# A chunk's second 64 outputs in exchanged halves of the partitions, so that the products with the states use all four quarters of TensorE's array

## What is computed

```python
for t in range(S):
    cur = np.einsum('bhd,bhe->bhde', u[None] * kt, vt)
    y[:, :, t] = np.einsum('bhd,bhde->bhe', rt, state + cur)
    state = wt[:, :, :, None] * state + np.einsum('bhd,bhe->bhde', kt, vt)
```

## Time and profile before

| | us |
|---|---|
| median of 3 runs (612.76 to 614.74) | 613.3 |
| the profiled execution | 613.21 |
| its span on the core | 611.5 |
| PE busy / DVE busy / ACT busy | 588.1 / 327.2 / 267.1 |
| PE busy from 85 to 510 us | 424.68 of 425 |

### The profile page before, as it was taken

The page is one execution under the profiler, slowest core; times in us unless marked ns, Lnnn a source line. Parts: engine busy times, 40 slices in busy tenths (PEclk is TensorE's granted clock), DMA queues, the critical chain, the costliest instruction groups (busy, mean ns, idle before and its releaser), DMA issues.

```text
span 611.5 us, 15134 instructions
## 1 busy us (share of the span) xinstructions
PE 588.1 (96%) x6342; PEld 526.4 (86%) x6342; DVE 327.2 (54%) x710; ACT 267.1 (44%) x540; POOL 12.4 (2%) x30
## 2 busy tenths in 40 slices
PE   7888989999999999999999999999999999999983
PEld 6787989899989999999899999999999999997433
DVE  8768675476755654566266635564455323323304
ACT  3845543544453344433543354335433346553314
POOL 4000000000000000000000000000000000000000
PEclk9989999999999999999999999999999999999996
DMA  8975602324402330333023312323031097667628
GB/s 292 348 229 174 183 25 77 101 62 117 124 18 86 100 101 1 101 88 88 29 62 100 101 41 61 83 67 93 2 101 28 14 366 266 218 228 277 230 82 309
DMA packets 46309, 77.50 MB, mean 127 GB/s; under 512 B 3296, under 2 KB 35040, under 8 KB 43664
## 3 DMA queue, kind: packets, MB, share of 16 engines
q1 hardware_dynamic: 45040, 71.80, 37.8%
q0 software_dynamic: 1200, 4.72, 2.5%
HBM read 67.46 MB, written 9.04 MB: 125 GB/s over the span
## 4 chain that ended last, share of the span: by engine, by line
PE 86%; DMA 6%; DVE 4%; issue 2%; ACT 1%; SPq 0%; DVEq 0%; ACTq 0%
PE hps L1262 32%; PE acc L1397 31%; DMA w2s<-w 2%; PE yps L1215 2%; PE mps L1293 2%; PE zps L1195 2%; PE mps L1469 2%; PE zps L1206 2%; DMA stage<-w_out 1%; PE zps L1215 1%; PE zps L1221 1%; DMA raw<-dmaj 1%; DMA out<-obuf 1%; PE mps L1482 1%; PE mps L1502 1%
## 5 line engine op out<-in xcount | busy, mean ns | idle before, releaser
L1102 DVE TENSOR_TENSOR gl<-g,gh 128x384 fp32r<-128x384 f32 (+1 forms) x144 | 74.0, 514 | 232.8 <-ACT gh L802 232.5
L1262 PE MATMUL hps<-xh,wi_hi 128*128 128x384 f32 (+1 forms) x432 | 147.7, 342 | 2.3 <-DVE xl L499 2.1
L1262 PE MATMUL hps<-xh,wi_lo 128*128 128x384 f32 (+1 forms) x432 | 137.3, 318 | 0.0
L1262 PE MATMUL hps<-xl,wi_hi 128*128 128x384 f32 (+1 forms) x432 | 137.3, 318 | 0.0
L1397 PE MATMUL acc<-wo_hi,gh 128*128 128x384 f32 x384 | 129.8, 338 | 0.6 <-ACT x L809 0.3
L1397 PE MATMUL acc<-wo_hi,gl 128*128 128x384 f32 x384 | 129.6, 338 | 0.0
L1397 PE MATMUL acc<-wo_lo,gh 128*128 128x384 f32 x384 | 129.6, 338 | 0.0
L802 ACT ACTIVATE gh<-g 128x384 fp32r<-128x384 f32 (+1 forms) x144 | 70.4, 489 | 130.8 <-PE acc L1397 130.4
L798 ACT ACTIVATE g<-hps 128x384 f32<-128x384 f32 (+1 forms) x144 | 65.7, 456 | 133.5 <-PE hps L1262 130.8
L1262 PEld LDWEIGHTS hps<-xh,wi_hi 128*128 128x128 f32 x432 | 81.4, 188 | 12.7 <-issue 6.6
L1262 PEld LDWEIGHTS hps<-xl,wi_hi 128*128 128x128 f32 x432 | 81.8, 189 | 0.9
(11 more groups left out here) (235 smaller groups left out, 733.8 us busy)
## 6 DMA issues: line engine op xcount, KB each, us to landing
raw<-dmaj SPq DMA_DIRECT2D x23, 903.0 KB, 5.6
w1s<-w SPq DMA_DIRECT2D x16, 768.0 KB, 6.4
w2s<-w SPq DMA_DIRECT2D x16, 768.0 KB, 6.3
vn<-vnat SPq DMA_DIRECT2D x24, 192.0 KB, 2.6
tests<-wall SPq DMA_DIRECT2D x6, 768.0 KB, 15.2
out<-obuf SPq DMA_DIRECT2D x12, 384.0 KB, 4.2
y_scratch<-ybuf SPq DMA_DIRECT2D x44, 96.0 KB, 2.0
x<-y_scratch SPq DMA_DIRECT2D x22, 192.0 KB, 2.5
```

Source lines behind the costliest of these rows:

```text
L1102: dve.tensor_tensor(out=gl[F % 2][:, 0:wide], in0=g32[F % 2][:, 0:wide], in1=gh[F % 2][:, 0:wide].bitcast(fp32), op=ALU.subtract).then_inc ...
L1262: last = pe.matmul(hps[F % 2][:, 0:wide], w[:, g, at:at + 128], v[i % 2][:, g, 0:wide], start=m == 0, stop=m == 3 * G - 1)
```

## The change

Results of the second 64 tokens (c = 1) go to the exchanged half of the partitions: head par 0 to partitions 64 to 111, par 1 to 0 to 47. `out_rows` gives the place. With it a `from_state` product takes quarter (par, par) for c = 0 and (par, 1 - par) for c = 1, and a `from_block` product (c, par) for c = 0 and (1, 1 - par) for c = 1. Since `ybuf` then holds the second 64 columns exchanged, all that reads or writes it goes by halves: the bonus sums (a second set of weights with exchanged columns, `heads_u[1]`, `headsum[1]`), the values (the host exchanges them in `dmaj`), the stores to DRAM (four DMAs of 64 columns for two of 128), `permute` (a second `place_rows`). Counts of semaphores follow. In `outputs` the order becomes: for each pair the two products whose result another quarter continues (`apart`), then the two others (`same`); then `from_block` of `same` for pair 0, the wait, and the rest.

```diff
+        def out_rows(c, par):
+
+            at = HALF * (par if c == 0 else 1 - par)
+            return slice(at, at + D)
...
                 for par in range(2):
-                    sp.dma_start(view[par], ybuf[n % 2][HALF * par:HALF * par + D]).then_inc(y_stored[n % 2], 16)
+                    for c in range(2):
+                        cols = slice(HALF * c, HALF * (c + 1))
+                        sp.dma_start(view[par][:, :, cols], ybuf[n % 2][out_rows(c, par), :, cols]).then_inc(y_stored[n % 2], 16)
...
-            pool.memset(place_rows[:, :], 0.0).then_inc(made, 1)
+            for c in range(2):
+                pool.memset(place_rows[c][:, :], 0.0).then_inc(made, 1)
...
-            for par in range(2):
-                rows = place_rows[HALF * par:HALF * par + D]
-                pool.affine_select(out=rows, in_=rows, compare_op=ALU.not_equal, fill=1.0, base=96 + D * par,
-                                   pattern=[[-1, 288]], channel_multiplier=1).then_inc(made, 1)
+            for c in range(2):
+                for par in range(2):
+                    rows = place_rows[c][out_rows(c, par)]
+                    pool.affine_select(out=rows, in_=rows, compare_op=ALU.not_equal, fill=1.0, base=96 + D * par,
+                                       pattern=[[-1, 288]], channel_multiplier=1).then_inc(made, 1)
...
-                for p in range(HP):
-                    last = act.activation(heads_u[p][:, :], headsum_f[:, :], ACT.Copy, scale=ucols[:, p:p + 1])
+                for c in range(2):
+                    for p in range(HP):
+                        last = act.activation(heads_u[c][p][:, :], headsum[c][:, :].bitcast(fp32), ACT.Copy,
+                                              scale=ucols[:, p:p + 1])
...
-            dve.tensor_copy(headsum[:, :], headsum_f[:, :])
+            dve.tensor_copy(headsum[0][:, :], headsum_f[:, :])
+            dve.tensor_copy(headsum[1][:, 0:D], headsum_f[:, HALF:R])
+            dve.tensor_copy(headsum[1][:, D:HALF], headsum_f[:, D:HALF])
+            dve.tensor_copy(headsum[1][:, HALF:R], headsum_f[:, 0:D])
...
-                    return pe.matmul((zps, yps)[c][rows, p * HALF:(p + 1) * HALF], (state[n % 2], midway)[c][rows, p, :],
+                    return pe.matmul((zps, yps)[c][out_rows(c, par), p * HALF:(p + 1) * HALF], (state[n % 2], midway)[c][rows, p, :],
...
-                for swap in (1, 0):
-                    for p in range(HP):
-                        for par in range(2):
-                            last = from_state((par + swap) % 2, par, p)
-                    if swap:
+                apart, same = ((0, 1), (1, 0)), ((0, 0), (1, 1))
+
+                for p in range(HP):
+                    for c, par in apart:
+                        last = from_state(c, par, p)
+                    if p == HP - 1:
                         last.then_inc(crossed, 1)
+                    for c, par in same:
+                        from_state(c, par, p)
+                for c, par in same:
+                    from_block(c, par, 0)
                 pe.wait_ge(crossed, n + 1)
                 for p in range(HP):
-                    for c in range(2):
-                        for par in range(2):
-                            last = from_block(c, par, p)
+                    for c, par in apart:
+                        last = from_block(c, par, p)
+                    if p + 1 < HP:
+                        for c, par in same:
+                            from_block(c, par, p + 1)
...
-                for g, p in ((0, 0), (0, 1), (1, 1), (1, 2), (2, 2), (2, 3)):
-                    at = 96 + 128 * g - 96 * p
-                    last = pe.matmul(hps[c][:, g * C:(g + 1) * C], place_rows[:, at:at + 128], ybuf[c][:, p, :],
-                                     start=p == g, stop=p > g)
+                for half in range(2):
+                    cols = slice(HALF * half, HALF * (half + 1))
+                    for g, p in ((0, 0), (0, 1), (1, 1), (1, 2), (2, 2), (2, 3)):
+                        at = 96 + 128 * g - 96 * p
+                        last = pe.matmul(hps[c][:, g * C + HALF * half:g * C + HALF * (half + 1)], place_rows[half][:, at:at + 128],
+                                         ybuf[c][:, p, cols], start=p == g, stop=p > g)
...
                 for p in range(HP):
-                    last = pe.matmul(bonus_bank(n)[0:R, p * C:(p + 1) * C], heads_u[p][:, :], ruk[n % 2][:, p, :],
-                                     start=True, stop=True)
+                    for c in range(2):
+                        last = pe.matmul(bonus_bank(n)[0:R, p * C + HALF * c:p * C + HALF * (c + 1)], heads_u[c][p][:, :],
+                                         ruk[n % 2][:, p, HALF * c:HALF * (c + 1)], start=True, stop=True)
...
-                        pe.matmul(mps[0:R, :], headsum[:, :], rukh[:, :, :].rearrange("d p t -> d (p t)"),
-                                  start=True, stop=False)
-                        pe.matmul(mps[0:R, :], headsum[:, :], rukl[:, :, :].rearrange("d p t -> d (p t)"),
-                                  start=False, stop=True).then_inc(u_done, 1)
+                        for c in range(2):
+                            cols = slice(HALF * c, HALF * (c + 1))
+                            sums = mps[0:R, :].rearrange("e (p t) -> e p t", p=HP)[:, :, cols]
+                            pe.matmul(sums, headsum[c][:, :], rukh[:, :, cols], start=True, stop=False)
+                            last = pe.matmul(sums, headsum[c][:, :], rukl[:, :, cols], start=False, stop=True)
+                        last.then_inc(u_done, 1)
```

More of the change, by code:

```diff
@@ L116, in attention_mlp_soft_experts @@
         headsum_f = sb("headsum_f", [R, R])
-        headsum = sb("headsum", [R, R], f32r)
+        headsum = [sb(f"headsum{c}", [R, R], f32r) for c in range(2)]
         ucols = sb("ucols", [R, HP])
@@ L132, in attention_mlp_soft_experts @@
         strip = place[0] - 2 * G * ST * 4 + 2 * C * 4
-        heads_u = [sb(f"heads_u{p}", [R, R], at=strip + (p + 1) * ST * 4) for p in range(HP)]
+        heads_u = [[sb(f"heads_u{c}{p}", [R, R], at=strip + (HP * c + p + 1) * ST * 4) for p in range(HP)] for c in range(2)]
         g32 = [sb(f"g32_{i}", [128, ST]) for i in range(2)]
         gh = [sb(f"gh{i}", [128, ST], f32r) for i in range(2)]
-        place_rows = sb("place_rows", [R, 288], at=place[0])
+        place_rows = [sb(f"place_rows{c}", [R, 288], at=place[0] + c * 288 * 4) for c in range(2)]
         gl = [sb(f"gl{i}", [128, ST], f32r) for i in range(2)]
@@ L405, in general_loads @@
                 for par in range(2):
-                    sp.dma_start(ybuf[n][HALF * par:HALF * par + D], view[par]).then_inc(gen_back, 16)
+                    for c in range(2):
+                        cols = slice(HALF * c, HALF * (c + 1))
+                        sp.dma_start(ybuf[n][out_rows(c, par), :, cols], view[par][:, :, cols]).then_inc(gen_back, 16)
         def split_x(act, i, c):
@@ L693, in _ @@
             pool.memset(ident[:, :], 0.0).then_inc(made, 1)
[L694 removed]
+            for c in range(2):
+                pool.memset(place_rows[c][:, :], 0.0).then_inc(made, 1)
             for q in range(EG):
                 pool.memset(sel[q][:, :, :], 0.0).then_inc(made, 1)
[L697 removed]
+            pool.wait_ge(made, 6 + EG)
             for c in range(2):
@@ L712, in _ @@
                 for j in range(4):
-                    pool.wait_ge(made, 10 + EG + 4 * q + j)
+                    pool.wait_ge(made, 13 + EG + 4 * q + j)
                     s0 = SPE * (4 * q + j)
@@ L1029, in start_up @@
                 products(0)
-                dve.wait_ge(made, 10 + EG)
+                dve.wait_ge(made, 13 + EG)
                 for m in range(3):
@@ L1318, in start_up @@
             def start_up():
-                pe.wait_ge(made, 10 + EG)
+                pe.wait_ge(made, 13 + EG)
                 pe.wait_ge(headsum_made, 1)
@@ L1592 @@
             dmaj[:, HALF * par:HALF * par + D, q, :, 1:] = by_feature(a)[:, par]
+    for par in range(2):
+        dmaj[:, HALF * par:HALF * par + D, VV, :, 1 + HALF:] = by_feature(v)[:, 1 - par, :, :, HALF:]
     ucol = np.zeros((R, HP), np.float32)
```

17 lines of the change are left out of this document (9 added, 8 removed).

## The result

| | before | after |
|---|---|---|
| median, us | 612.76 (7 runs, 611.89 to 614.74) | 617.47 (7 runs, 615.62 to 622.83) |
| the profiled execution, us | 613.21 | 615.69 |
| its span, us | 611.5 | 614.0 |
| PE busy / DVE busy / ACT busy, us | 588.1 / 327.2 / 267.1 | 591.9 / 327.2 / 268.3 |

The changed kernel is slower: its time over that of before is 1.0088, with a 95% interval of 1.0067 to 1.0109. The forecast was 614.6 us with a range that ended at 617.5, so the time lies just inside its end, and "slower by over 0.3%" had 0.41. Run again beside other kernels, the same file gave 617.63 us against 613.18 (1.0109, 1.0072 to 1.0147).

What follows compares the result with a forecast made beforehand. PE was taken to bound 85 to 510 us, and one PE, DVE and ACT chain the start-up; 613.2 + 4.05 (start-up) + 0.7 (chunk 3 sums) - 0.2 (later sums) - 3.15 (`outputs`) gave 614.6 us, range 610.0 to 617.5.

Steps and rivals of the forecast that it cites:

- The outputs: In `outputs`, first to last start falls from 1.33 to 1.18 us: 0.15 us gained a chunk, 3.15 us for 21 chunks.
- Rival (A): In `outputs`, two row halves writing one PSUM bank take turns, so it lasts 1.56 us: 623.0 us; chance 0.07.
- Rival (C): In `outputs`, the wait for `crossed` costs nothing, so the gain is the full 0.41 us a chunk: 608.9 us; chance 0.05.
- (D): In the stores, packets of 256 bytes take twice the time, `x` comes late and ACT stands: about 617.5 us; chance 0.06.
- The narrow products with full weights: In `permute` and `bonus_sums`, weight loads set the step, so half-width passes cost +1.3 us per `permute`, +0.7 per sums.
- Rival (B): In `permute` and the bonus sums, weight load is not the limit and half the width costs half: 610.1 us; chance 0.08.
- The start-up up to `xh`: Start-up chain through the second `permute`: 0.9 + 0.7 + 1.3 - 0.15 + 1.3 = 4.05 us later.
- So the shift is whole: At the start-up's end, the first slot waits for ACT's tests, so all 4.05 us of delay carries through.
- the sums of chunk 3: Bonus sums in the start of the steps: not hidden by any PE wait, +0.7 us.
- the sums of chunk 2: Bonus sums in step 0: their +0.7 us is hidden by PE's waits of 0.29 and 0.88 us for DVE.
- The sum: Whole kernel, against the profiled 613.2 us: + 4.05 + 0.7 - 0.2 - 3.15 = +1.4, so 614.6 us.
- the sums of the later chunks: Head sums as four products of 256 columns for two of 512: 0.46 us for 0.47, -0.2 us over 20 chunks.

Runs made afterwards that it cites:

- sums_away: The changed kernel with the second head-sum matrix (`headsum[1]`) allocated behind all other buffers, so every other buffer lies where it lay before; measured 617.82 us.

## Why the prediction was wrong, point by point

The forecast was 1.4 us more than before and the medians are 4.7 us apart. Three things make the difference: where the new buffer lies, which the sum didn't have; how much of the start-up's cost reaches the end, which it had too high; and executions at a lower clock, which it didn't have.

**The outputs**: right. The gain was forecast as 0.15 us a chunk with a wait of 0.30 us; it is 0.178 with a wait of 0.28 to 0.29. That is 21 x 0.03 = 0.6 us more than in the sum, inside its bounds.

**Rival (A)**, two row halves in one bank: ruled out. Four passes start every 0.056 us in `from_state` after the change, with both row halves writing into `zps` and both into `yps`. The rule of the Trainium skill that was weighed there (TensorEngine Tiling (Array Packing), Gotcha 1: PSUM Pressure) is not borne out where the two write different partitions. Rival (C), a wait that costs nothing, falls by the gap from 138.54 to 138.70; (D) by `x`, which still lands in a median of 2.5 us, with the stores at 1.7 for 2.0:

```profile
y_scratch<-ybuf SPq DMA_DIRECT2D x88, 48.0 KB, 1.7
x<-y_scratch SPq DMA_DIRECT2D x22, 192.0 KB, 2.5
```

**The narrow products with full weights**: right. The weights set the step, not the width: 0.113 us for `permute` (0.114 forecast), 0.10 us for the sums ((1.78 - 0.27) / 15 in the rows above, 0.098 forecast). Rival (B) falls.

**The start-up up to `xh`**: 3.93 us for 4.05 forecast, though not link by link: `score` came 0.47 us later and the sums of chunk 0 cost 0.7, those of chunk 1 next to nothing.

**"So the shift is whole"**: the first step that failed. Of 3.93 us at 28 us only 2.42 were left at the first mark (95 us), where the sum had 4.75 with the sums of chunk 3, less 0.15 for that chunk's outputs. Where it went, the starts of the same product with `w_in` before and after show: the first one starts 3.93 us later after the change, the first behind PE's branch at the start-up's end 3.17. The branch had more idle time before than after:

```profile
34.55 0.39 PE L1372 MATMUL acc<-warm 128*128 128x256 f32 x1 [1.43 <-issue]
```

```profile
37.73 0.39 PE L1398 MATMUL acc<-warm 128*128 128x256 f32 x1 [0.69 <-issue]
```

Behind the sums of chunk 2 the shift is 3.46 us, and some ten us of PE's work later it is 1.49. Before:

```profile
48.30 0.36 PE L1262 MATMUL hps<-xh,wi_hi 128*128 128x256 f32 x1
...
60.00 0.37 PE L1262 MATMUL hps<-xh,wi_hi 128*128 128x256 f32 x1
```

After:

```profile
51.76 0.36 PE L1285 MATMUL hps<-xh,wi_hi 128*128 128x256 f32 x1
...
61.49 0.36 PE L1285 MATMUL hps<-xh,wi_hi 128*128 128x256 f32 x1
```

Between these two lie PE's waits of 0.29 and 0.88 us for DVE; neither is in the profile after. The prediction let them swallow the 0.7 us of the sums of chunk 2 and nothing else. The stretch swallowed 1.97 us: their 1.17, the 0.18 won in the outputs of chunk 2, and some 0.6 that I can't assign. Of the 2.2 us that the sum has too much up to the first mark, 0.74 are the branch's and 1.27 this stretch's. I asked of ACT and the first slot whether they had slack, and not of the slots behind.

The profiled execution of before had a stretch at a low clock right there, which the profile after doesn't have:

```profile
36.00:40.00 4.00, 4.00 (x20) 4.00 (x19) 4.00 (x5) 2.62 (x5) 0.49 (x1) 0.57 0.91 238
```

It isn't what makes the shift small: none of the profiles of the other kernels with this start-up has such a stretch, and their first marks lie on both sides of its 95.33 us (94.69 to 96.37).

**"The sum"**: the second step that failed, and the dear one. Between the marks the forecast has 19 x 0.15 + 0.2 = 3.05 us of gain; they show 0.31. The term that is missing is where the new matrix lies: nothing in the sum asked what it does to the buffers behind it. Its price is 2.9 us in the kernel before and 3.1 us (386.49 - 383.39) in the changed one, 0.5 of it in the sums of the later chunks, which the prediction had at -0.2 us and which took 0.67 more. In the profiled execution, +1.4 us forecast and +2.5 measured, the errors nearly cancel, which is luck: 4.6 - 2.4 = 2.2 us too much up to the first mark, 3.05 - 0.31 = 2.7 too little between the marks, and behind the second, where the sum had a gain of 0.15, 0.4 us of loss, 0.5 too little.

**The clock**: what the profiled execution could not show. The forecast took the median to lie where the profiled execution lay, as before the change (0.1 us). After it the median is 1.8 us above, since some executions are 4 to 8 us longer at a lower mean clock, and the runs with parts of the change put this on the halved permutes. One row of before bears on it, and I passed over it: right behind the branch it has already a stretch at a low clock (the row of 36 to 40 us above).

So the mechanism in `outputs` was read rightly, and so was the price of the narrow products in `permute` and in the sums of chunk 0. What failed is what becomes of a cost on its way to the end, and a cost that no instruction carries. With 64 bytes more behind the new matrix the changed kernel takes 613.71 us, 0.9 us from the forecast, and that nearness is luck in part: all but one of its executions at a clock of 0.991 and above took some 3 us less than forecast, the others up to 4 more.

## What to carry to other kernels

A gain inside a steady loop and a cost in the start-up should be timed apart: limit the change to the chunks that have it cheap (here chunks 4 to 23) before giving it up, and follow a shift through every later wait until it has met all the slack. When an edit adds or resizes a buffer, run a control that adds the buffer alone: here 448 unused bytes cost nearly the whole gain, and 64 more gave it back. And compare many executions, not one profile, where the edit changes what TensorE does in the start-up: here a stretch at half the clock put the first mark 3.3 us back (101.09 for 97.75), nearly what the edit wins.

## What the runs showed of the hardware that I had not expected

- Where the moving and the weight operands of the wide fp32r products begin in a partition changes their pace: 386.80 us between two marks with a start at 64 or 320 bytes behind a multiple of 512, 387.57 at 128, 389.73 on the multiple itself. Of these last 2.93 us 1.44 are in products whose weights were moved and 1.26 in products whose streamed operand was.
- Passes of different row halves that write different partitions of one bank don't disturb each other: 0.056 us a step in each of four quarters.
- A wide product between narrow ones costs both ways: 0.14 us into it and 0.32 us out of it (with PE's own wait behind it), for a step of 0.12 us among its like.
- A product of PE that waits for another of PE's own starts 0.28 to 0.29 us behind the start of that one's last pass, which itself lasts 0.22 us.
- TensorE stayed at 1.2 GHz for 10 us of the start-up while it had work throughout (10.50 us busy of 10.50; the profile of sums_away, with a mean clock of 0.978). Other executions of that kernel had a mean clock of up to 0.992, and the profiles of the changed kernel, with the same start-up, have no such stretch.
